# Attention with a computed bias, then a gated MLP: preparing the first two head pairs at other places of the bias stage

## What is computed

```python
B, H, S, D = 4, 8, 576, 64
scores = (1 / sqrt(D)) * q @ k^T
psi_rel = log1p(abs(i - j));  psi_i = log1p(max(i, 1))
x = (psi_rel / psi_i)[..., None]
bias = relu(x @ w1 + b1) @ w2            # 32 hidden features, 8 heads
attn = softmax(scores + bias)            # row maximum subtracted, 1e-9 added to the sum
x = (attn @ v) as [2304, 512]
out = (sigmoid(x @ w_gate) * (x @ w_val)) @ w_out      # 512 -> 1536 -> 512
```

## Time and profile before

| | us |
|---|---|
| median of 3 runs | 801.66 |
| lowest, highest | 801.59, 801.71 |
| the profiled execution | 801.59 |
| its span, first to last instruction | 799.7 |
| bias stage: first feats to the last copy of sums | 5.6 to 64.6 |
| step 0: first score matmul | 64.7 |
| step 5: first score matmul | 81.5 |

### The profile page before, as it was taken

How to read it: one execution, slowest core, us unless ns; L and a number is a source line. 1 busy time by engine, 2 the same in 40 slices (tenths; PEclk the granted TensorE clock), 3 DMA queues, 4 the chain that set the end, 5 groups by cost and what they waited for, 6 DMA issues and landing times.

```text
span 799.7 us, 13831 instructions
## 1 busy us (share of the span) xinstructions
PE 769.3 (96%) x5296; PEld 638.9 (80%) x5296; DVE 349.1 (44%) x845; ACT 344.7 (43%) x684; POOL 194.7 (24%) x363
## 2 busy tenths in 40 slices
PE   6777999999999999999799999999999999999998
PEld 2335777777777777789789998999899899989996
DVE  6995777777777777522511220222022112201220
ACT  6996767667777667621412221222122112202210
POOL 0002666556545557768000000000000000000000
PEclk9998999999999999999999999999999999999999
DMA  5879243332423322133211000100200020000001
GB/s 130 192 188 204 71 105 82 80 93 68 124 68 75 80 74 69 55 93 119 80 66 54 1 0 27 53 1 14 66 0 1 14 66 1 1 26 14 1 1 39
DMA packets 86337, 49.92 MB, mean 62 GB/s; under 512 B 60161, under 2 KB 79745, under 8 KB 86273
## 3 DMA queue, kind: packets, MB, share of 16 engines
q1 hardware_dynamic: 86272, 49.05, 23.5%
HBM read 28.98 MB, written 9.44 MB: 48 GB/s over the span
## 4 chain that ended last, share of the span: by engine, by line
PE 85%; DMA 4%; DVE 4%; ACT 2%; POOL 2%; SPq 1%; issue 1%; POOLq 0%; ACTq 0%; DVEq 0%
PE f_ps L1052 18%; PE g_ps L998 16%; PE u_ps L998 16%; PE v_ps L978 11%; PE so_ps L914 8%; PE ty_ps L927 4%; PE tx_ps L939 3%; DVE feats L719 3%; DMA x_raw<-in_w_out 2%; PE so_ps L909 2%; PE so_ps L859 1%; SPq L382 1%; POOL w L523 1%; PE tx_ps L956 1%; PE v_ps L872 1%
## 5 line engine op out<-in xcount | busy, mean ns | idle before, releaser
L998 PE MATMUL g_ps<-x_h,w 128*128 128x384 f32 x576 | 147.9, 337 | 3.9 <-DVE hid L828 3.9
L998 PE MATMUL u_ps<-x_h,w 128*128 128x384 f32 x576 | 146.5, 335 | 0.0
L828 DVE TENSOR_TENSOR hid<-u_ps,sig 128x384 f32<-128x384 f32 x72 | 40.1, 557 | 239.5 <-PE u_ps L998 239.5
L613 ACT ACTIVATE probs<-neg_scores,neg_max 128x576 f32<-128x576 f32 x144 | 111.1, 772 | 59.0 <-DVE neg_max L750 59.0
L506 POOL TENSOR_SCALAR probs<-probs,recip 128x512 f32<-128x512 f32 x128 | 88.6, 693 | 160.8 <-DVE recip L770 160.8
L998 PEld LDWEIGHTS g_ps<-x_h,w 128*128 128x128 f32 x576 | 104.7, 189 | 5.0 <-DVE hid L828 4.2
L998 PEld LDWEIGHTS u_ps<-x_h,w 128*128 128x128 f32 x576 | 104.1, 188 | 0.5 <-issue 0.5
L681 ACT ACTIVATE h_h<-hid 128x384 fp32r<-128x384 f32 x72 | 37.8, 526 | 149.6 <-DVE hid L828 149.6
L998 PE MATMUL g_ps<-x_l,w 128*128 128x384 f32 x288 | 97.1, 337 | 0.0
L998 PE MATMUL u_ps<-x_l,w 128*128 128x384 f32 x288 | 96.3, 334 | 0.0
L750 DVE CUSTOM_DVE_ANT_0 neg_scores<-so_ps,bias 128x576 f32<-128x576 f32 x128 | 91.9, 756 | 4.8 <-PE so_ps L914 3.8
(11 more groups left out here) (84 smaller groups left out, 1133.5 us busy)
## 6 DMA issues: line engine op xcount, KB each, us to landing
bias<-bias_rows SPq DMA_DIRECT2D x12, 576.0 KB, 6.1
x_raw<-attn_transposed SPq DMA_DIRECT2D x6, 768.0 KB, 4.6
out<-out_sb SPq DMA_DIRECT2D x18, 256.0 KB, 2.0
q_raw<-in_q SPq DMA_DIRECT2D x32, 128.0 KB, 2.6
k_raw<-in_k SPq DMA_DIRECT2D x32, 128.0 KB, 2.5
v_main<-in_v SPq DMA_DIRECT2D x32, 128.0 KB, 2.3
w_raw<-in_w_gate SPq DMA_DIRECT2D x12, 256.0 KB, 3.0
w_raw<-in_w_val SPq DMA_DIRECT2D x12, 256.0 KB, 2.9
```

Source lines behind the costliest of these rows:

```text
L613: nc.scalar.activation(probs[s % RING][:, place, :], neg_scores[:, place, :], ACT.Exp, bias=neg_max[:, stat(s, place)], scale=-1.0, accum_ ...
L828: nc.vector.tensor_tensor(hid[f % 2][:, :], u_ps[f % 3][:, 0:CH], sig[f % 2][:, :], ALU.mult).then_inc(gated, 1)
L998: last = nc.tensor.matmul(bank[f % 3][:, 0:CH], w[:, f, part, i, t, :], x[:, t, :], start=m == 0, stop=m == len(terms) - 1)
```

## The change

The preparation of pair 0 is no longer spread over units 6, 8 and 10. PE turns q, tails and k one after another ahead of unit 6, ACT makes the three high parts behind the copy of unit 5, and DVE the three low parts behind the features of unit 6. The preparation of q of pair 1 moves from step 2 into the bias stage: PE turns it ahead of unit 18, into `tx_ps` and no longer into `v_ps`, ACT copies it behind the copy of unit 17, DVE subtracts behind the features of unit 18. SP's load of q of pair 2 moves from step 3 to a place between the stores of duos 10 and 11. And `last_rows` lies under `neg_scores` and no longer under `probs2`; `neg_scores` is first written in step 0, so the shift of step 0 now waits for the last store from that buffer, duo 15.

```diff
-TAILS_UNIT = 8
-KEYS_UNIT = 10
+SECOND_UNIT = 18
...
-        probs = [sb(f"probs{i}", [P, 2, S]) for i in range(RING - 1)]
+        probs = [sb(f"probs{i}", [P, 2, S]) for i in range(RING)]
+
+        prob_tails = [sb(f"prob_tails{i}", [P, 2, REM]) for i in range(RING)]
         with ExitStack() as bias_only:
             last_rows = sb("last_rows", [P, 2, S], F32, bias_only)
-        probs.append(sb(f"probs{RING - 1}", [P, 2, S]))
-
-        prob_tails = [sb(f"prob_tails{i}", [P, 2, REM]) for i in range(RING)]
         neg_scores = sb("neg_scores", [P, 2, S])
...
+        def q_turned_ps(pair):
+
+            return tx_ps[:, 0:NT * P] if pair == 1 else v_ps[:, 0:NT * P]
...
+                if d == SECOND_UNIT // 2 + 2:
+                    sp.wait_ge(q_turned, 2)
+                    load_q(2)
                 store_bias(d)
...
-                if s == 3:
-                    sp.wait_ge(q_turned, 2)
-                    load_q(2)
...
             for u in range(UNITS):
-                if u == PREP_UNIT + 1:
+                if u == PREP_UNIT:
                     high_q(0)
-                if u == TAILS_UNIT + 1:
                     high_tails(0)
-                if u == KEYS_UNIT + 1:
                     high_k(0)
+                if u == SECOND_UNIT:
+                    high_q(1)
                 if u + 1 < UNITS:
                     relu_feats(u + 1)
                 copy_bias(u)
...
-                if s == 2:
-                    high_q(1)
...
-                        to = ROW_STEP if s == 0 else DUOS
+                        to = ROW_STEP if s == 0 and d < ROW_BUFS - 1 else DUOS
...
             for u in range(UNITS):
-                if u == PREP_UNIT + 3:
+                if u == PREP_UNIT + 1:
                     low_q(0)
-                if u == TAILS_UNIT + 3:
                     low_tails(0)
-                if u == KEYS_UNIT + 3:
                     low_k(0)
+                if u == SECOND_UNIT + 1:
+                    low_q(1)
                 max_feats(u)
...
-                elif pair >= 1:
-                    pe.wait_ge(q_low, pair)
-                to = v_ps[:, 0:NT * P]
+                elif pair == 2:
+                    pe.wait_ge(q_low, 1)
+                to = q_turned_ps(pair)
...
                 else:
+                    pe.wait_ge(q_low, 2)
                     pe.wait_ge(tails_low, 2)
...
                 if u == PREP_UNIT:
                     pe.wait_ge(ident_ready, 3)
                     turn_q(0)
-                if u == TAILS_UNIT:
                     turn_tails(0)
-                if u == KEYS_UNIT:
                     turn_k(0)
+                if u == SECOND_UNIT:
+                    turn_q(1)
                 bias_unit(u)
...
-                    if s == 2:
-                        turn_q(1)
```

More of the change, by code:

```diff
@@ L587, in high_q @@
                     act.wait_ge(scored, SPP * (pair - 1) - 1)
-                nc.scalar.activation(qk_h[pair % 2][:, Q_MAIN:], v_ps[:, 0:NT * P], ACT.Copy).then_inc(q_high, 1)
+                nc.scalar.activation(qk_h[pair % 2][:, Q_MAIN:], q_turned_ps(pair), ACT.Copy).then_inc(q_high, 1)
             def high_k(pair):
@@ L724, in low_q @@
                 dve.wait_ge(q_high, pair + 1)
-                nc.vector.tensor_tensor(qk_l[pair % 2][:, Q_MAIN:], v_ps[:, 0:NT * P], plain(qk_h[pair % 2][:, Q_MAIN:]),
+                nc.vector.tensor_tensor(qk_l[pair % 2][:, Q_MAIN:], q_turned_ps(pair), plain(qk_h[pair % 2][:, Q_MAIN:]),
                                         ALU.subtract).then_inc(q_low, 1)
@@ L795, in _ @@
                     move_b(s - LAG)
-                if s == 2:
-                    low_q(1)
                 if m == 4 and pair + 2 < PAIRS:
```

## The result

The changed kernel takes **807.1 us** (median of six executions, 806.6 to 808.1) where the kernel before takes 801.6 on the same chip (six, 800.0 to 802.9): the ratio is 1.0069, 95% interval 1.0058 to 1.0081. The forecast was 805.1 with a range of 803.0 to 806.6. The direction was right and most of the mechanism too; the time lies 2.0 us above the forecast and 0.5 above the range, so the sum was wrong in size.

The account below looks back on a forecast made before the run. PE was taken to bound the kernel, with DVE pacing the bias stage and late stores deciding step 2. Step 2's shift +3.72 and its exponential -0.25 made +3.47 on 801.66: 805.1 us, range 803.0 to 806.6.

Parts of the forecast that it names:

- What bounds the kernel: Whole kernel: PE bound, 96% busy; the change only moves the start of step 5's scores, after which both kernels run alike.
- Part 1: Bias stage, pair 0's block at unit 6: DVE idles 1.11 us waiting for ACT's high part; +0.92 us net.
- part 2: Bias stage, q of pair 1 at unit 18: 1.10 idle plus 0.60 low part, +1.70 us, partly falling into slack.
- Part 2's -0.5: Behind unit 25: ACT's waits of 0.27 and 0.36 us for old stores go, -0.5 us (bounds 0 and -0.63).
- part 3: Step 0's shift waits for duo 15's store, landing at 70.4 us, 1.25 of it the load; shift +4.67 us.
- Rival (d): Load of q of pair 2 costs double for its 256-byte rows: landing at 71.7 us, 806.3 us in all; chance 0.06.
- rival (a): Duo 15's store lands in time, so the first shift waits for nothing: 802.6 to 803.6 us; chance 0.17.
- Rival (c): Not slower: store queue drained and clock up over scores 1 and 2, 801.1 us; chance 0.07.
- The start of the queue: Store queue behind the tail stores: said to begin later by part 1's 0.92 us, moving duo 15's landing by that.
- Part 4: Step 2's shift: the old wait of 0.95 us for the last stores is swallowed, leaving +3.72 us.
- Part 5: Step 2 without its preparation of q: ACT's high part no longer delays the exponential, -0.25 us.
- The sum: Whole kernel: 3.72 - 0.25 = +3.47 us on 801.66, giving 805.1 us; the forecast's chance was 0.50.

Follow-up runs that it names:

- x14: The changed kernel run again without an edit, its second trace: ratio 1.0058 to the kernel before.
- x15: The changed kernel run once more without an edit, its third trace: ratio 1.0065 to the kernel before.
- x4: The kernel before with only q of pair 1 prepared at unit 18, the load of q of pair 2 still at step 3: ratio 0.9999.
- x9: The changed kernel with the load of q of pair 2 back at step 3 and the negated scores at their old place: ratio 1.0026 to the kernel before.
- x1: The changed kernel with the negated scores at their old place (last_rows under the third probs buffer): ratio 1.0053 to the kernel before.
- x7: The changed kernel with 15 filler PE transposes ahead of unit 7 and of unit 19: ratio 1.0062 to the kernel before.
- x13: The changed kernel with the eight small tail stores of duo 9 issued by GpSimd instead of SP: ratio 1.0085 to the kernel before.
- x2: The kernel before with only the new place: last_rows under neg_scores, step 0's shift waiting for duo 15's store: ratio 1.0026.
- x3: The kernel before with only pair 0 prepared in one block at unit 6: ratio 1.0022.
- x6: The changed kernel with ACT's high parts one unit later and DVE's low parts two: ratio 1.0074 to the kernel before.
- x17: x6 run again, second trace: ratio 1.0065 to the kernel before.
- x10: The changed kernel with the load of q of pair 2 between the small tail stores of duos 8 and 9: ratio 1.0085 to the kernel before.
- x12: The kernel before with the eight small tail stores of duo 9 issued by GpSimd instead of SP: ratio 1.0052.

## Why the prediction was right and wrong

**What bounds the kernel** held: the rest behind scores 5 is unchanged to 0.1 us, and PE is without a gap through the attention stage. The MLP stage has two, in both kernels, and with them and the clock there the rest differs by up to 1.9 us among the 16 traces.

**Part 1** (+0.92) and the first half of **part 2** (+1.70) held where the clock stayed up: 1.02 and 1.82, with waits of 1.13. Missing was that behind the gap which they leave on PE the clock can fall, 0.93 to 1.15 each. "PE's part is hidden behind DVE" looked at the order of work and not at the speed of what follows. By x14 against x15 this explains the late bias stage of the first trace, and only in part the time, if at all.

**Part 2's -0.5 failed.** The waits on old buffers go when stores move by less than the copies do, and x4 and x9 show it (units 25 to 35 in 14.70, -0.78). In the changed kernel these units take 15.57 and 15.74 in two traces (14.69 in the third) against 15.48, because the load, which I counted only in part 3, stands ahead of duo 11's store on SP and gives ACT a new wait of 0.96. The change's own DMA was moved past a queue whose next entry I didn't look at.

**Part 3, the landing of duo 15's store, is the step that failed, and in it the load is the term that was mis-sized.** I divided bytes by the mean rate of the stretch: 1.25. Measured are 1.9 us at duo 15's landing by the means (0.1 to 2.1 by single pairs of traces) and 2.2 at the shift of step 2 (x1 against x9). Rival (d) came as near with 2.5, for another reason, the small rows. The row by which I saw no surcharge for small rows doesn't decide that: in the stretch of 210 GB/s, too, 2216 of 3831 packets are under 512 B. What the issue does could have been read from the trace of the kernel before. Its timeline of SP has the same two DMAs for q of pair 1 behind a bias store, and two later loads of q:

```profile
24.79 0.53 SPq L376 DMA_DIRECT2D bias<-bias_rows  x1
25.37 2.64 SPq L344 DMA_DIRECT2D q_raw<-in_q  x2
...
76.06 1.06 SPq L344 DMA_DIRECT2D q_raw<-in_q  x2
...
80.71 0.92 SPq L344 DMA_DIRECT2D q_raw<-in_q  x2
```

Behind a store of 576 KB issued 0.6 us ahead they hold SP for about 2.6, elsewhere for about 1. But hold and price aren't the same: between x9 and x1 duo 11's store is issued 2.83 us later and lands 1.4 later, of which the 1.25 by bytes would be most. I did not vary the rows' size or the hold alone, so how much is bytes and how much issue stays open. The mechanism itself, the first shift waiting for duo 15's store, was right, and so was the rejection of rival (a): of the traces with the new place and the load, only x7 and x13 have the store in time for the first shift, and there ACT had waited for a buffer until then. Rival (c) appears in no trace.

**The start of the queue** was the second miss in the same part. I let the landing move by part 1's 0.92. The tail stores follow copy 17, which moved by 1.01 (x14) to 1.95 (changed), and 2.12 in x15. The landing, counted from copy 5, moved by 4.1, 3.1 and 3.4 us in the three traces where 2.17 was forecast.

**Part 4** held: step 0's shift to step 2's takes 7.04 to 7.05 us in all three traces of the change (forecast 60.01 - 53.10 = 6.91), so the slack of 0.95 was swallowed as said. In x2, too, 2.14 at the first shift leave 1.33 at step 2. **Part 5** held: from step 2's shift to scores 5 the changed kernel takes 7.68, before 7.90: -0.22 for -0.25. Where the lower clock reaches over the scores of step 3 this is lost (7.86 in x14, where the low level lasts 10.2 us and not the 6.8 of before).

**The sum** was +3.47. Scores 5 came 5.74, 4.88 and 4.99 later in the three traces. At the least disturbed of them, x14, what is missing is 1.41: 0.9 more at the landing of duo 15, 0.14 in the ring of steps 0 and 1, 0.2 of clock at step 3, and 0.16 between that landing and the shift. The ratios put the whole at 4.7 to 5.5.

**What stays open**: executions of one kernel spread by 1.5 to 7 us in this study (the kernel before 799.7 to 804.6 on one chip). One such execution in a trace differs from the next by where the clock falls, by how long duo 11's store takes (7.0 us in the changed kernel, about 9 in x7) and by PE's waits in the MLP stage; what makes them differ I could not show. None of the versions beat the kernel before: the only one that can't be told from it is x4.

## To carry to other kernels

When a change moves a DMA in among large stores, look in the trace of before for how long the same DMA holds the issuing queue in such a place, and at who is next in that queue, as well as at its bytes; here 256 KB cost about 2 us instead of 1.25 behind a large store, and less amid the small ones. When a tile is laid over another buffer, look for the landing of that buffer's last store and ask first whether the stores or the engines decide the step; once the stores do, what is won or lost behind the start of their queue changes little (x4), while what puts that start off, as the block does, is still paid (x3). Put two hand-overs between engines a unit or more apart: in a block the first of them costs a wait, here 1.1 us, and behind the gap that it left on PE the clock fell in four of ten traces.

## What the runs showed of the hardware

- **Behind one and the same gap the clock falls in some executions and not in others.** Behind the same idle of 2.09 us PE's granted clock fell to 0.50 in four of ten traces, behind 1.89 in two of ten, and behind 1.93 of x6 and x17 in one of two. The Trainium skill, page TensorE: Matmul & The Clock Gate, section A second HAM failure mode: psum-queue depth-cycling, describes a kernel in which PE pauses briefly and often and the clock swings between its two levels. No run here tells that cause from another.
- **A load can hold its issuing queue.** The two DMAs of 128 KB took 0.58 and 1.95 us to issue behind a store of 576 KB (0.59 and 2.01 in the kernel before, at 25.37), 0.99 together amid the tail stores. The share of the DMA engines doesn't tell the two places apart beforehand: it is 0.53 in 52 to 53 us of the changed kernel and in 44 to 45 us of x10, where these loads begin.
- **Small stores from GpSimd among SP's large ones land late.** The DMA view of x12, from 38 to 60 us, has them at a median of 6.4 us (3.6 to 10.5); the landings of the same stores issued by SP are not in the records:

```profile
bias_tail<-bias_rows POOLq DMA_DIRECT2D x8, 72.0 KB, 6.4
```
